# Filler matmuls at three waits, the zeros of a scatter target in four transfers, and a reordered GpSimd queue

## The reference

```python
# attention: q, k, v are (2, 8, 576, 64)
q_d = q.reshape(B, H, Sd, 4, D).mean(axis=3)       # k_d, v_d alike
out_up = np.repeat(sm_attn(q_d, k_d, v_d), 4, axis=2)
scores = np.where(|i - j| < 4, scale * q @ k.T, -1e9)
x = out_up + softmax(scores) @ v                    # -> 1152 tokens x 512
# experts, 8 of them with room for 288 tokens each
expert_idx = np.argmax(x @ w_gate, axis=1)
disp[e, counts[e]] = x[i]                           # in order of tokens
y = relu(disp @ w1) @ w2                            # 512 -> 1024 -> 512
x = gate_w[i] * y[expert_idx[i], pos[i]]
# last layer, 512 -> 2048 -> 512
h = x @ w_in
out = (h * tanh(softplus(h))) @ w_out
```

## Time and profile before

| | |
|---|---|
| median of 3 runs | 474.72 us (471.12 to 475.45) |
| the profiled execution | 477.65 us |
| its span, first to last instruction | 475.5 us |
| mean granted clock of TensorE | 0.968 |
| TensorE busy | 447.9 us, 94% of the span |
| VectorE, ScalarE, GpSimd busy | 59%, 48%, 29% |
| chain that ended last | PE 84%, DVE 6%, ACT 4%, issue 3%, DMA 1% |

### The profile page before, as it was taken

The page is one execution under the profiler, slowest core; times in us unless marked ns, Lnnn a source line. Parts: engine busy times, 40 slices in busy tenths (PEclk is TensorE's granted clock), DMA queues, the critical chain, the costliest instruction groups (busy, mean ns, idle before and its releaser), DMA issues.

```text
span 475.5 us, 10038 instructions
## 1 busy us (share of the span) xinstructions
PE 447.9 (94%) x3380; PEld 412.8 (87%) x3381; DVE 280.7 (59%) x665; ACT 230.1 (48%) x631; POOL 137.2 (29%) x136
## 2 busy tenths in 40 slices
PE   8869898989879999999999999999999999999993
PEld 7658687878879999999999898899988999988982
DVE  7879577679202102102111599888888888888873
ACT  2756665642313323332223566655665655656541
POOL 9587325111000000000004455433253333433202
PEclk9979899599989999999999999999999999999998
DMA  9999999232867988996846234123141121321001
GB/s 186 196 193 152 166 379 347 101 112 74 293 240 243 357 300 281 350 311 207 281 159 207 82 88 45 43 88 90 44 143 57 49 83 45 90 110 44 1 0 66
DMA packets 72143, 74.97 MB, mean 158 GB/s; under 512 B 32816, under 2 KB 47920, under 8 KB 72112
## 3 DMA queue, kind: packets, MB, share of 16 engines
q1 hardware_dynamic: 70384, 69.84, 51.0%
q0 software_dynamic: 1728, 4.72, 2.6%
HBM read 65.11 MB, written 9.44 MB: 157 GB/s over the span
## 4 chain that ended last, share of the span: by engine, by line
PE 84%; DVE 6%; ACT 4%; issue 3%; DMA 1%; SPq 1%; POOLq 0%; POOL 0%; ACTq 0%; DVEq 0%
PE ps L1174 79%; ACT pr L703 2%; PE ps L1256 2%; PE ps L1421 1%; DMA qk_tok<-in_q 1%; PE ps L1302 1%; SPq L431 1%; DVE mx L928 1%; DVE sme L935 1%; PE ps L1251 0%; DVE qT L901 0%; ACT prT L686 0%; DVE kdT L887 0%; DVE qdT L887 0%; DVE gL L1080 0%
## 5 line engine op out<-in xcount | busy, mean ns | idle before, releaser
L637 POOL TENSOR_TENSOR wiL<-raw,wiH 128x512 fp32r<-128x512 f32 x48 | 62.5, 1303 | 251.5 <-ACT wiH L686 148.3
L1174 PE MATMUL ps<-xe,raw 128*128 128x128 f32 (+2 forms) x512 | 71.7, 302 | 4.7 <-issue 3.9
L1174 PEld LDWEIGHTS ps<-xe,raw 128*128 128x128 f32 x512 | 70.4, 194 | 5.6 <-issue 4.4
L1174 PE MATMUL ps<-hid,raw 128*128 128x128 f32 (+2 forms) x512 | 70.8, 297 | 0.0
L1174 PEld LDWEIGHTS ps<-hid,raw 128*128 128x128 f32 x512 | 69.0, 191 | 0.0
L1174 PE MATMUL ps<-x2H,wiH 128*128 128x384 f32 x192 | 65.1, 339 | 0.3 <-DVE x2L L1080 0.3
L1174 PE MATMUL ps<-x2L,wiH 128*128 128x384 f32 x192 | 65.3, 340 | 0.0
L1174 PE MATMUL ps<-x2H,wiL 128*128 128x384 f32 x192 | 64.6, 337 | 0.0
L1174 PE MATMUL ps<-woH,gH 128*128 (+1 forms) x144 | 56.9, 395 | 2.5 <-DVE gL L1080 2.5
L1174 PE MATMUL ps<-woH,gL 128*128 (+1 forms) x144 | 57.2, 397 | 0.0
L1174 PE MATMUL ps<-woL,gH 128*128 (+1 forms) x144 | 56.7, 394 | 0.0
(11 more groups left out here) (140 smaller groups left out, 769.1 us busy)
## 6 DMA issues: line engine op xcount, KB each, us to landing
raw<-in_moe_w SPq DMA_DIRECT2D x32, 1024.0 KB
raw<-in_moe_w_in SPq DMA_DIRECT2D x24, 512.0 KB
x_by_expert<-x_sb SPq DMA_DIRECT2D x1, 4608.0 KB, 15.5
xg<-x_by_expert SPq DMA_DIRECT2D x8, 512.0 KB, 3.6
wo_in<-in_moe_w_out SPq DMA_DIRECT2D x8, 512.0 KB
v<-in_v SPq DMA_DIRECT2D x4, 576.0 KB
qk_tok<-in_k SPq DMA_DIRECT2D x8, 256.0 KB, 4.8
qk_tok<-in_q SPq DMA_DIRECT2D x8, 256.0 KB, 5.1
```

The costliest lines, as they stand in the source:

```text
L637: nc.gpsimd.tensor_tensor(wiL[:, r, :, :], raw_wi_tile(r), wiH[:, r, :, :].bitcast(F32), ALU.subtract).then_inc(s_wil, 1)
L1174: return T.matmul(out_, a, b, start=start, stop=stop, skip_group_check=True)
```

## The change

Four edits. (1) Three fills of 16 filler matmuls in turns of 4, each put ahead of a wait: before the scores of step 4 and ahead of its wait for the pooled q and k; in round 3 before the transposes of the probabilities of step 2, ahead of the wait for their scaling; in round 8 ahead of the product of pooled step 6. The other turns are shortened (10 to 5, 8 to 4) at unchanged totals. (2) The zeros go in four transfers of 576 rows, each from 96 partitions with 6 rows apiece. The first stands where the one stood; the others are issued behind local 2, 3 and 4. (3) The four weight units are issued behind local 1, 3, 5 and 6. (4) On GpSimd the placing of pooled steps 4 and 5 comes between `sum_v(2)` and `sum_v(3)`.

```diff
-TURN_LOADS, TURN_DOWN, TURN_LOCAL = 10, 8, 6
+TURN_LOADS, TURN_DOWN, TURN_LOCAL, TURN_WAIT = 5, 4, 6, 4
+WARM_SUMS, WARM_NORM, WARM_PROBS = 16, 16, 16
+ZERO_PARTS, ZERO_P = 4, 96
+UNIT_BEHIND = {1: 0, 3: 1, 5: 2, 6: 3}
+ZERO_BEHIND = {2: 1, 3: 2, 4: 3}
@@ SyncE
-            sp.dma_start(xe_dram[0:E * CAP, :].rearrange("(p a) d -> p a d", p=P),
-                         x_sb[:, NT - 1, :].unsqueeze(1).to_broadcast([P, E * CAP // P, DM])).then_inc(s_zf, 16)
+            def zero_rows(i):
+                rows = E * CAP // ZERO_PARTS
+                per = rows // ZERO_P
+                sp.dma_start(xe_dram[i * rows:(i + 1) * rows, :].rearrange("(p a) d -> p a d", a=per),
+                             x_sb[0:ZERO_P, NT - 1, :].unsqueeze(1).to_broadcast([ZERO_P, per, DM])).then_inc(s_zf, 16)
+            zero_rows(0)
-            for i in range(4):
-                sp.wait_ge(s_av, RANK[local_step(i if i < 3 else KEPT - 1)] + 1)
-                load_unit(0, i)
+            for t in range(1, 7):
+                sp.wait_ge(s_av, RANK[local_step(t)] + 1)
+                if t in UNIT_BEHIND:
+                    load_unit(0, UNIT_BEHIND[t])
+                if t in ZERO_BEHIND:
+                    zero_rows(ZERO_BEHIND[t])
@@ GpSimd
-            for j in range(KH, B * KH):
-                sum_v(j)
+            sum_v(KH)
+            pool.wait_ge(s_vd, KH + 1)
+            place_od(FIRST_DOWN[0])
+            place_od(FIRST_DOWN[0] + 1)
+            sum_v(KH + 1)
             pool.wait_ge(s_vd, B * KH)
-            for n in range(NS):
+            for n in range(FIRST_DOWN[0] + 2, NS):
                 if is_down(n):
                     place_od(n)
-            pool.wait_ge(s_zf, 16)
+            pool.wait_ge(s_zf, 16 * ZERO_PARTS)
@@ ScalarE, x_copy
-                    act.wait_ge(s_zf, 16)
+                    act.wait_ge(s_zf, 16 * ZERO_PARTS)
@@ TensorE, probs_t
+                if n >= 1:
+                    pe.wait_ge(s_ptc, n)
+                if n == HELD - 2:
+                    keep_warm_in_turns(6, WARM_NORM, TURN_WAIT)
                 if down:
                     pe.wait_ge(s_exp, n + 1)
                 else:
                     pe.wait_ge(s_nrm, sum(STEPS[m][0] == "local" for m in range(n + 1)))
-                if n >= 1:
-                    pe.wait_ge(s_ptc, n)
@@ TensorE, the rounds
+                    if n == FIRST_DOWN[0]:
+                        keep_warm_in_turns(2 * (n % 2), WARM_SUMS, TURN_WAIT)
                     if n in FIRST_DOWN:
                         pe.wait_ge(s_qd, HELD + 1 if n == FIRST_DOWN[0] else NT)
+                if n == local_step(HELD) + 1:
+                    pe.wait_ge(s_kTc, NT)
+                    keep_warm_in_turns(TB, WARM_PROBS, TURN_WAIT)
                 for m in attended(n):
                     if m == n - 2:
                         attend(m)
```

## The result

The changed kernel took 476.50 us (median of 20 runs, 471.68 to 482.35) against 474.29 us of the kernel before (20 runs): a ratio of 1.0053, 95% interval 1.003 to 1.0076. Forecast was 469.8 us, and the range ended at 475.0. It is slower by about half a per cent, some 2.5 us, and not faster by 1%.

What follows compares the result with a forecast made beforehand. TensorE (84% of the chain's last engine) was taken as the bound, with clock drops in the first 105 us. Gains 2.0 + 0.5 + 0 + 2.4 = 4.9 us, from 474.72 to 469.8 us; range 464.8 to 475.0.

Steps and rivals of the forecast that it cites:

- The zeros: Four parts; last lands 4.5 us after issue behind local 4, scatters begin at 82.7 instead of 78.94; cost nothing.
- third drop: TensorE at half clock from about 83.2 to 96.8 us; moves one round later, so one round runs full clock: 2.4 us.
- The fills: Fillers in TensorE's waits keep the clock up: 2.0 us from rounds 3 and 4, 0.5 us from the third.
- first drop: TensorE falls to 1.2 GHz at 28.8 us after idle waits; two fills there bring 2.0 us.
- third fill: Ahead of pooled step 6's product, in a 1.43 us wait with 0.16 to spare: adds 0.5 us (bounds 0 and 1.4).
- second drop: TensorE falls to 1.2 GHz at about 52.4 us after waiting for ScalarE's copy; local 0's product and following scores lose 1.4 us.
- GpSimd's order: Placings of steps 4 and 5 before `sum_v(3)` end at about 48.6, not 50.1; local 0 wants 50.7: gives 0.
- The rivals: Stall and third drop gone 465.9 (0.25); third stretch unshortened 472.2 (0.20); nothing 474.7 (0.09); slower 480.0 (0.08).
- a loop that stalls on its code: Slower rival: one of three added TensorE loops stalls 3.63 us, then a clock drop; 5.3 us, 480.0 us, chance 0.08.

Runs made afterwards that it cites:

- e2: Kernel before with only the four zero transfers and the later weight units: ratio 1.0044 to the kernel before.
- g2: Kernel before with only the weight units moved, behind local 1, 3, 5 and 6; zeros in one transfer: ratio 0.9965.
- h1: Changed kernel with the zeros in one transfer again, all else kept: 469.82 us against 470.6 for the kernel before, ratio 0.9935.
- g1: Kernel before with only the four zero transfers, behind local 2, 3 and 4; weight units where they were: ratio 1.0104.
- e6: e1 with its one zero transfer taken from 96 partitions with 24 rows each instead of 128 with 18: one execution timed, 476.63 us.
- e8: Changed kernel again, unaltered, on another chip: ratio 1.0063 to the kernel before.
- e1: Changed kernel with zeros (one transfer) and weight units put back, leaving fills and GpSimd's order: ratio 0.9944 to the kernel before.
- e5: Changed kernel with the last three zero parts issued one round earlier, behind local 1, 2 and 3: ratio 1.003 to the kernel before.
- g3: e2 with every zero part but the first one round later, behind local 3, 4 and 5: ratio 1.0117 to the kernel before.
- e3: e1 with each of the first six scatters issued only when the one before has landed: ratio 1.0169 to the kernel before.
- f4: f3 with the second and third zero part issued behind local 1 and 2: ratio 1.0008 to the kernel before.
- f3: Changed kernel with zeros in three parts from 128 partitions instead of four from 96, the last still behind local 4: ratio 1.0166 to the kernel before.
- f2: e1 again, unaltered, on another chip: ratio 1.0008 to the kernel before.
- h2: e1 a third time, unaltered, beside h1: ratio 0.9995 to the kernel before.
- e7: e1 with a fourth fill of 16 fillers in round 8, ahead of local 0's wait for its windows of v: ratio 0.9997 to the kernel before.
- f1: Kernel before with the three fills and their turns alone; GpSimd's order, zeros and units as before: ratio 0.9978.
- e4: e1 with units 0 and 1 behind local 1 and 3, units 2 and 3 after expert 0's first rows are fetched: ratio 0.9992 to the kernel before.

## Why the prediction was wrong, point by point

**The zeros, costed at nothing: the step that failed.** The prediction let the fourth part land 4.5 us after its issue, with bounds 3.9 and 6.5, and went on: the scatters begin at 82.7 in old time, and none of the six that must land before the early rows are fetched becomes late. The cost was to be 0. What the runs showed in its place: with all else alike, the split zeros cost 0.8% (e2 against g2) and 1.2% (the changed kernel against h1), 3.7 and 5.6 us, as differences of ratios from different chips; quotients of medians give 0.5% and 0.6%. By themselves they cost 1.0% (g1).

The first mistake is the landing. The last part took 8.2 us in the changed kernel, and 7.4 to 11.8 us in all six profiles with four parts, beyond the upper bound. In the changed kernel the third part was still in flight until 81.4 us, and weight unit 2 was issued beside the last at 80.1. That the 96 partitions add to it is likely from e6, but no run shows it for a part by itself. So the scatters began at 86.3 to 87.7 us (after, e8).

The second mistake was to compare the scatters only with the release of their rows. Six of them, 1.27 us apart, end 7.6 us after the first begins; the next thing in the chain, the fetch of the first rows for expert 0, then waits for the last of them to land. In e2 the sixth started at 91.24 us and the first rows were in SBUF at 98.6; in e1 at 89.73 and 96.0. TensorE was ready about 96.5. The prediction had this cover in its hands (early rows wanted from 105 us in the old trace) but measured it on an execution that the third drop had made late, and its own forecast moved TensorE's need forward by 4.9 us without moving the supply. The wait that this gives is 1.96 us in e5, 2.08 in e2, 2.43 in e8, 3.28 in g1 and 8.62 in g3, and 7.58 in e3, where the paced scatters make it and the zeros are early. It is absent in all other profiles: those with one zero transfer, f4, and the two (after, f3) in which the zeros were late but a stall and half clock made TensorE later still.

Set beside each other, most of the kernels took longer the later the zeros were complete (in the one profile of each):

| kernel | zeros complete, us | ratio |
|---|---|---|
| with the fills: h1, e1, f2, h2 | 70.9 to 72.1 | 0.9935, 0.9944, 1.0008, 0.9995 |
| f4 | 76.2 | 1.0008 |
| e5 | 81.3 | 1.0030 |
| f3 | 81.9 | 1.0166 |
| changed kernel, e8 | 85.4, 86.8 | 1.0053, 1.0063 |
| without the fills: g2 | 71.8 | 0.9965 |
| e2 | 83.7 | 1.0044 |
| g1, g3 | 92.9, 94.5 | 1.0104, 1.0117 |

Two things stay open. f3 is out of line. And in e2 the wait is 2.08 us, while the zeros cost 3.7 there by the ratios and 2.4 by the medians; whether and where a rest goes isn't shown. Half clock at the first rows doesn't settle it, since h1 has that too (94.7 to 101.6 us). That zeros and units together cost less (1.0044) than the zeros alone (1.0104) fits with unit 3 standing ahead of the last part in g1, but the two ran on different chips.

**The fills.** Their mechanism was right where the first drop is concerned: it is in all five profiles without the fills (from 27.9 to 29.0 us) and in none of the fourteen with them, and the fillers of round 5 came 2.6 us earlier against 2.4 forecast. The third fill ends just as the product of pooled step 6 starts in the profile after (45.73 + 1.28 and 47.03), so its cover was used up; that cost nothing, as local 0 waited further on. Their worth was over-sized: 2.5 us forecast, about 1 us measured, not clear of nothing (0.9944, 1.0008, 0.9995, and 0.9978 without the order). The prediction took the second part of the cover from GpSimd and ScalarE, and overlooked the loads of v: local 0 also waits for the last window of batch 0, which lands at 50.8 us in the trace after and at 51.3 in that of before. In every profile with the fills but e7 local 0 started 0.2 us behind that landing, at 50.17 to 52.40 us, and the fills did not bring that landing forward (51.3 before, 50.0 to 52.2 with them). In that wait the clock may fall again, as it did in the changed kernel, in e6 and in e8. The second drop was a matter of the execution before the change too: of the kernels without fills it is absent in e2 and g2. The one profile with a fourth fill (e7) has no second drop, but neither have ten of the thirteen that have three fills alone, and it gained nothing.

**GpSimd's order.** Cost and gain 0 forecast, and that held. In f1 the old order ended the second placing at 50.81 us (50.1 forecast), and the windows, at 51.90, were last. Should the windows come earlier, the old order would hold local 0 back in f1 by 0.35 us at most (TensorE was ready at 50.46). That the view names GpSimd as the releaser there is its way with a wait for several semaphores, and the landing events correct it.

**The third drop, 2.4 us.** The forecast was one round at full clock in place of half; in the profile after the half clock lasted 17.1 us, against 13.6 before. This term rested on one execution. The stall with remote releasers (2.7 us or more) stands in the profiles of before, after, f1, f2, f3 and f4, and not in the thirteen others, among them e1 and h2, which are f2's own kernel, and e8, which is that of after. So the kernel alone does not make it. Whether the chip does can't be told from the execution: all four profiles of the chip of f1 to f4 have it, and none of the thirteen of the four other chips of the experiments. In all six it lies within the burst of the first scatters. A unit in flight beside the scatters is not enough for it (e2 and e8 had both), and e3 and e4 could not test its cause, as e1 did not show it. One thing more sets the same six apart: their traces lack 91 to 156 landing events of transfers, the thirteen others at most 5. After has 2506 and e8, the same kernel, 2662; f2 has 2517 and e1 and h2, the same kernel, 2614 each. A stall in which records get lost may belong to the taking of the profile and not to the kernel; no run decides it. f2's profiled execution, with the stall, took 468.01 us, where the median of its runs is 473.26. What makes it stays open. A term that one execution shows, and that no structure of the program makes necessary, should not have been 2.4 of 4.9 us.

**The rivals.** The one with opposite sign, a loop that stalls on its code, did not occur: in no profile does a filler loop start behind a gap that has no other releaser. By the Trainium skill ("Runtime: NRT & Kernel Launch", Instruction fetch mechanics) a taken branch to code outside the window that is held forces a fetch. These loops jump back a few instructions, and the profiles agree: they show no such stall at them. What did go the other way, zeros late and with them expert 0's first rows, was not among the rivals, although the prediction worked through each of its links.

## What to carry to other kernels

When a transfer is delayed because there is slack, follow the chain to its last consumer and set every link at the new times, those that the rest of the change brings forward included: here zeros, six scatters in a row, their landing, the fetch, TensorE. Do not go from 128 partitions to 96 only to make the rows divide: the whole transfer took 23.0 us instead of 15.4 to 16.3 (e6). A stall seen in one profile needs a second profile of the same kernel, on another chip too, before it becomes a term of a sum. And where an engine waits for several semaphores, set the releaser that the view names beside the landings: in f1 it named GpSimd, and a load of v was last.

## What the runs showed of the hardware

The same 4.5 MB written from SBUF with 2 KB rows took 15.4 to 16.3 us from 128 partitions (ten profiles) and 23.0 us from 96 (e6, one execution). The 16 engines' ends were 0.8 us apart in the kernel before and 8.8 us in e6, with three weight units issued meanwhile in both.

Scatters of GpSimd issued while a weight unit was landing moved their first bytes only behind most of it. The kernel before shows it, and so does e2, whose scatters started at 84.59 us with unit 2 in flight until 87.1. From 86 to 88 us its hardware queue moved 0.71 MB and the scatters' queue nothing; from 88 to 90 us the scatters' queue moved 0.52 MB.

In six of nineteen profiles ScalarE or VectorE stood still for 2.7 to 5.8 us during the first scatters with no releaser in the trace, and the same six lack landing events. The same kernel has this in one profile and not in another, and no run shows whether it also happens when no profile is taken.
